# Attention and two mixture-of-experts layers in one kernel: other routing one-hots and ranks, one table of rows, another order of the attention loads

## The reference

```python
# attention: B 4, H 8, S 768, D 64; block 32, window 16
k_sum = k.reshape(B, H, nb, block, D).max(axis=3)
v_sum = v.reshape(B, H, nb, block, D).mean(axis=3)
scores_l = scale * q @ k^T         # kept where |i - j| < 16
scores_s = scale * q @ k_sum^T + log(32)
a = softmax(concat(scores_l, scores_s))
attn = a @ concat(v, v_sum)        # -> x: 3072 tokens of 512
# first expert layer: 8 experts, 512 -> 1024 -> 512
do = x @ w_skip > 0                # the others pass unchanged
e = argmax(x @ w_gate);  g = softmax prob of e
x[do] += g * (relu(x @ w1[e]) @ w2[e])
# second expert layer: the same sizes, each expert takes exactly 384 tokens
# all (token, expert) logits in falling order: a pair is taken if the token
# is free and the expert has room
out[mask_e] = relu(x[mask_e] @ w1[e]) @ w2[e]
```

## Time and profile before

| | us |
|---|---|
| median of 3 runs | 919.61 (914.32 to 926.02) |
| the profiled execution itself | 920.52 |
| its span, first to last instruction | 918.8 |
| mean granted TensorE clock | 0.920 |

### The profile page before, as it was taken

The page is one execution under the profiler, slowest core; times in us unless marked ns, Lnnn a source line. Parts: engine busy times, 40 slices in busy tenths (PEclk is TensorE's granted clock), DMA queues, the critical chain, the costliest instruction groups (busy, mean ns, idle before and its releaser), DMA issues.

```text
span 918.8 us, 14353 instructions
## 1 busy us (share of the span) xinstructions
PE 769.8 (84%) x4727; PEld 524.7 (57%) x4727; DVE 388.0 (42%) x1530; ACT 220.5 (24%) x685; POOL 185.6 (20%) x236
## 2 busy tenths in 40 slices
PE   2788888877079999994329999999999999999995
PEld 1788888877057777682225454454545545555552
DVE  4585767845602121113763636346363553620000
ACT  2666667754001111010001011110111101111110
POOL 4472736323021111111010020111101011031101
PEclk8898999989579999997558999999999999999998
DMA  8999795999073518600050330504205050155000
GB/s 187 201 244 227 183 244 129 244 254 293 13 280 130 194 58 322 246 7 7 1 218 1 126 127 1 218 34 164 88 10 208 35 218 35 53 220 197 35 0 34
DMA packets 137827, 126.02 MB, mean 137 GB/s; under 512 B 100722, under 2 KB 100722, under 8 KB 137584
## 3 DMA queue, kind: packets, MB, share of 16 engines
q1 hardware_dynamic: 125584, 94.74, 34.1%
q10 hardware_dynamic: 6432, 14.73, 5.6%
q0 software_dynamic: 5760, 15.87, 4.6%
HBM read 105.80 MB, written 22.74 MB: 140 GB/s over the span
## 4 chain that ended last, share of the span: by engine, by line
PE 66%; DVE 10%; DMA 9%; issue 5%; POOL 5%; SPq 2%; ACT 1%; POOLq 1%; DVEq 0%; ACTq 0%
PE bank L1085 19%; PE bank L1098 13%; PE bank L978 8%; PE bank L993 8%; DMA scratch<-rows_b,idx 4%; PE bank L1026 3%; DMA weights<-in_k 3%; PE bank L868 3%; PE bank L847 2%; POOL weights L626 2%; PE bank L1046 1%; PE bank L1058 1%; PE bank L857 1%; POOL scratch L657 1%; PE bank L890 1%
## 5 line engine op out<-in xcount | busy, mean ns | idle before, releaser
L1085 PE MATMUL bank<-scratch,weights 128*128 128x384 f32 x512 | 183.6, 503 | 0.7 <-ACT scratch L1261 0.7
L1098 PE MATMUL bank<-weights,scratch 128*128 128x512 f32 x384 | 178.8, 610 | 5.0 <-issue 2.5
L1085 PEld LDWEIGHTS bank<-scratch,weights 128*128 128x128 f32 x512 | 94.2, 192 | 59.7 <-issue 5.8
L1098 PEld LDWEIGHTS bank<-weights,scratch 128*128 128x128 f32 x384 | 70.3, 193 | 79.2 <-issue 76.4
L1167 ACT ACTIVATE scratch<-shared,neg_max 128x120 f32<-128x120 f32 x192 | 73.4, 383 | 45.6 <-DVE neg_max L1316 30.9
L1267 ACT ACTIVATE scratch<-bank 128x384 f32<-128x384 f32 x64 | 31.4, 490 | 171.1 <-PE bank L1085 171.1
L657 POOL TENSOR_TENSOR scratch<-scratch,row_inv 128x480 f32<-128x480 f32 x48 | 47.3, 986 | 99.2 <-DVE row_inv L1326 98.5
L978 PEld LDWEIGHTS bank<-mix,weights 128*128 128x128 f32 x512 | 60.6, 196 | 4.6 <-issue 4.6
L978 PE MATMUL bank<-mix,weights 128*128 128x128 f32 x512 | 61.5, 279 | 0.9 <-DVE mix L1522 0.9
L868 PE MATMUL bank<-shared,mix 120*128 120x128 f32 x384 | 53.2, 283 | 6.3 <-issue 6.3
L993 PE MATMUL bank<-weights,mix 128*128 128x512 f32 x128 | 58.4, 599 | 0.0
(11 more groups left out here) (234 smaller groups left out, 971.0 us busy)
## 6 DMA issues: line engine op xcount, KB each, us to landing
weights<-in_moe_w SPq DMA_DIRECT2D x20, 2048.0 KB, 11.6
scratch<-in_moe_w SPq DMA_DIRECT2D x8, 2048.0 KB, 15.6
weights<-in_moe_w ACTq DMA_DIRECT2D x16, 512.0 KB, 6.6
mix<-in_v SPq DMA_DIRECT2D x40, 192.0 KB
rows_a<-row SPq DMA_DIRECT2D x24, 260.5 KB, 4.1
rows_b<-row SPq DMA_DIRECT2D x24, 260.0 KB, 4.4
weights<-in_k SPq DMA_DIRECT2D x24, 256.0 KB, 5.6
scratch<-in_q SPq DMA_DIRECT2D x24, 256.0 KB, 4.8
```

Of the source, the lines that this page charges most:

```text
L1085: last = mm(hb2[f % 2][:, 0:CAP], w1_sb[odd][:, c, f * P:(f + 1) * P], xT2[odd][:, c, :], start=(c == 0), stop=(c == C - 1), skip_group_ch ...
L1098: last = mm(yb2[c % 2][:, :], hT2[odd][:, f, c * P:(c + 1) * P], w2_sb[odd][:, f, :], start=(f == 0), stop=(f == FC - 1), skip_group_check ...
```

## The change

- Each key tile has a semaphore of its own in every batch. SP's opening order is another: queries 3 after the first queries are turned and ahead of the means; the key tiles of batch 1 between windows. Keys of batch b + 2 are issued in tile steps 2, 3, 4, 4, 5, 5 of batch b.
- In odd steps the key turn follows the scores.
- The block means of batch 0: group 0 in five halvings on DVE after the key maxima, group 1 on POOL. In later batches POOL's fold starts a step earlier, its first halving is split over two steps, and the value block pieces are issued in steps 6 to 13 of the batch two before (before: 4 to 11).
- The quarters of the weights are issued in steps 39 to 46, one per step.
- One table `rows` of 529 columns (8 logits, 512 values, 9 logits) takes the place of both.
- First routing: tiles 0 to 22 are judged before the last tile's logits are copied; ranks over tiles come from 25 accumulating products; all one-hots have 16-bit operands and the tile index innermost. POOL loads one bound instead of nine and issues the first gather from the list itself.
- Second routing: the tokens of the closing expert are found from smaller operands, the updates of scores and assignments move behind the list's operands, the row one-hot is laid out in pairs of tiles, and `spacing` is another.

```diff
-            sp.wait_ge(s.v_sum_out, 16)
-            load_means(0)
-            load_means(1)
-            for g in range(2, VR, 2):
-                load_k(1, g - 2)
-                load_k(1, g - 1)
-                load_window(g)
-                load_means(g)
-                load_window(g + 1)
-                load_means(g + 1)
-            sp.wait_ge(s.q_turned, 1)
-            load_queries(3)
-            for j in range(TB - 2, TB):
-                load_k(1, j)
+            load_k(1, 0)
+            load_window(2)
+            sp.wait_ge(s.q_turned, 1)
+            load_queries(3)
+            sp.wait_ge(s.v_sum_out, 16)
+            for g in range(3):
+                load_means(g)
+            load_k(1, 1)
+            for g in range(3, VR):
+                load_window(g)
+                load_means(g)
+                load_k(1, g - 1)
+            load_k(1, TB - 1)
...
                 if b + 2 < B:
-                    sp.wait_ge(s.k_turned, TB * (b + 1))
-                    load_k(b + 2, w)
+                    for j in ((), (), (0,), (1,), (2, 3), (4, 5))[w]:
+                        sp.wait_ge(s.k_turned, TB * b + j + 1)
+                        load_k(b + 2, j)
...
+            FOLDS = 5
+            pool.wait_ge(s.blocks_in0, 16)
+            for step in range(FOLDS):
+                fold(0, step, slice(1, 2))
+            average(0, slice(1, 2))
             edges(0)
...
-                    at_ = n - (5 if b == 0 else 4)
+                    at_ = n - (4 if b == 0 else 3)
                     if at_ == 0:
                         pool.wait_ge(blocks_in[(b + 1) % 2], blocks_count(b + 1))
-                        fold(b + 1, 0)
+                        fold(b + 1, 0, slice(0, 1))
                     elif at_ == 1:
-                        fold(b + 1, 1)
-                        fold(b + 1, 2)
+                        fold(b + 1, 0, slice(1, 2))
                     elif at_ == 2:
-                        fold(b + 1, 3)
-                        fold(b + 1, 4)
-                        average(b + 1)
+                        fold(b + 1, 1, slice(0, 2))
                     elif at_ == 3:
+                        for step in range(2, FOLDS):
+                            fold(b + 1, step, slice(0, 2))
+                        average(b + 1, slice(0, 2))
...
-            mm(ranks[:, 0:NT * E], before[:, :], chosen_h.rearrange("p j e -> p (j e)"), start=True, stop=True)
-            mm(sums[:, 0:NT * E], ones[:, :], chosen_h.rearrange("p j e -> p (j e)"), start=True,
-               stop=True).then_inc(s.ranked_ps, 1)
+            mm(ranks[:, 0:(NT + 1) * E], before[:, :], chosen_h.rearrange("p j e -> p (j e)"), start=True, stop=False,
+               skip_group_check=True)
+            for j in range(NT):
+                last = mm(ranks[:, (j + 1) * E:(NT + 1) * E].rearrange("p (j e) -> p j e", e=E), ones[:, :],
+                          chosen_h[:, j:j + 1, :].to_broadcast([P, NT - j, E]), start=False,
+                          stop=(j == NT - 1), skip_group_check=True)
...
-                        last = mm(tot[:, 96:96 + 2 * CT], row_hot[:, :, j],
+                        last = mm(tot[:, 96:96 + 2 * CT], row_hot[:, j // 2, :, j % 2],
...
-            spacing = [20, 5, 10, 5] + [14, 5] * (ROUNDS - 2) + [13, 13, 11, 20]
+            spacing = [18, 7, 8, 7] + [12, 8] * (ROUNDS - 2) + [15, 11, 8, 17]
...
+                after = g - PIECES_AT          # 6
+                if 0 <= after and after // NH + 2 < B and after % NH < PIECES:
...
+                if QUARTERS_AT <= g < QUARTERS_AT + 2 * C:          # 39
...
-                v_.tensor_tensor(out=low_hot, in0=iota_row[:, :].rearrange("p (o n) -> p o n", o=1).to_broadcast([P, NT, P]),
-                                 in1=lo_f.rearrange("p (j o) -> p j o", o=1).to_broadcast([P, NT, P]), op=ALU.is_equal)
+                wide = [P, P, NT]
+                v_.tensor_tensor(out=low_hot, in0=iota_low[:, :, :],
+                                 in1=lo_h.rearrange("p (o j) -> p o j", o=1).to_broadcast(wide), op=ALU.is_equal)
...
+            link(judge(0, NT - 1))
+            copy_logits(NT - 1)
+            judge(NT - 1, NT).then_inc(s.phase_ready, 1)
+            copy_gates(NT - 1)
+            v_.memset(tile_bounds[:, 0:1], 0)
+            dve.wait_ge(s.ranked_ps, 1)
...
-                plink(v_.scalar_tensor_tensor(out=scores2, in0=over_experts(taken), ...
-                plink(v_.tensor_tensor(out=assigned, in0=assigned, in1=hot, op=ALU.add))
-                list_tokens(plink, ph, last_e)
+                plink(v_.tensor_tensor(out=mine_h, in0=taken, in1=here_h, op=ALU.mult))
+                plink(v_.tensor_tensor(out=mine_h, in0=mine_h, in1=kept_h, op=ALU.add))
...
+                list_tokens(plink, ph, update)
```

More of the change, by code:

```diff
@@ L262, in build @@
         first = sb("first", [P, NT])[:, :]
-        chosen = part(NT, E)
-        chosen_h = part(NT, E, dt=BF16)
-        prefix = part(NT, E)
-        tile_sum = [part(NT, E) for _ in range(2)]
-        count = part(E)
+        chosen_h = part(NT + 1, E, dt=BF16)
         over = part(E, NT)
@@ L392, in build @@
         at[0] = 0
-        xg2 = [part(CT, BROW) for _ in range(2)]
+        xg2 = [part(CT, ROW) for _ in range(2)]
         xT2 = [part(C, CAP) for _ in range(2)]
@@ L616, in _, with fold @@
             nc.gpsimd.memset(masks[:, 2, WK - WINDOW:WK], -1e30).then_inc(s.masks_made, 1)
-            v_links = [2]
-            def fold(b, step):
+            v_links = [0]
+            def fold(b, step, groups):
                 x = v_blocks[b % 2]
@@ L625, in fold @@
                 for lo in range(0, half, piece):
-                    last = nc.gpsimd.tensor_tensor(out=x[0:HB, :, lo:lo + piece], in0=x[0:HB, :, lo:lo + piece],
-                                                   in1=x[0:HB, :, half + lo:half + lo + piece], op=ALU.add)
+                    last = nc.gpsimd.tensor_tensor(out=x[0:HB, groups, lo:lo + piece], in0=x[0:HB, groups, lo:lo + piece],
+                                                   in1=x[0:HB, groups, half + lo:half + lo + piece], op=ALU.add)
                 last.then_inc(s.v_chain, 1)
@@ L902, in _ @@
                 kk = prepared(g)
-                if kk is not None:
+                if kk is not None and g % 2 == 0:
+                    pe.wait_ge(s.kT_vector, k_vector(kk))
+                    pe.wait_ge(s.kT_scalar, k_scalar(kk))
+                    turn_k(kk, kx)
+                if g + 2 < HT:
+                    score(g + 2)
+                if kk is not None and g % 2 == 1:
                     pe.wait_ge(s.kT_vector, k_vector(kk))
@@ L1383, in _ @@
             for g in range(HT + 2):
-                kk = prepared(g)
-                if kk is not None and kk % 2 == 0:
-                    put_k(kk, bank[7])
                 if g + 2 < HT:
@@ L1392, in _ @@
                     put_pT(g)
+                kk = prepared(g)
+                if kk is not None and kk % 2 == 0:
+                    put_k(kk, bank[7])
                 if 1 <= g <= HT:
@@ L1436, in running @@
                 return bufs[cur]
-            ranks, sums, table = bank[0], bank[1], bank[2]
-            def places(wait):
-                dve.wait_ge(s.ranked_ps, wait)
-                t3 = "p (j e) -> p j e"
-                link(v_.tensor_copy(tile_sum[0], sums[:, 0:NT * E].rearrange(t3, e=E)))
-                incl = running(link, tile_sum, NT, lambda x, a_, b_: x[:, a_:b_, :])
-                v_.tensor_copy(count, incl[:, NT - 1, :])
-                link(v_.tensor_tensor(out=place, in0=incl, in1=sums[:, 0:NT * E].rearrange(t3, e=E), op=ALU.subtract))
-                link(v_.tensor_tensor(out=place, in0=place, in1=ranks[:, 0:NT * E].rearrange(t3, e=E), op=ALU.add))
@@ new lines, in _, with judge @@
+            ranks, table = bank[0], bank[2]
+            def judge(a_, b_):
+                n = b_ - a_
+                experts = [P, n, E]
+                score = logits[:, a_:b_, 1:]
+                dve.wait_ge(s.logits_kept, b_)
+                v_.tensor_scalar(is_do[:, a_:b_], logits[:, a_:b_, 0], 0.0, None, ALU.is_gt)
+                link(v_.tensor_reduce(best[:, a_:b_], score, AX, ALU.max))
+                v_.tensor_scalar(none_at[:, a_:b_], is_do[:, a_:b_], -1.0, 4096.0, ALU.add, ALU.mult)
+                link(v_.tensor_tensor(out=equal[:, a_:b_, :], in0=score,
+                                      in1=best[:, a_:b_].rearrange("p (j o) -> p j o", o=1).to_broadcast(experts),
+                                      op=ALU.is_equal))
+                link(v_.tensor_tensor(out=equal[:, a_:b_, :], in0=equal[:, a_:b_, :],
+                                      in1=descend[:, :].rearrange("p (o e) -> p o e", o=1).to_broadcast(experts),
+                                      op=ALU.mult))
+                link(v_.tensor_reduce(first[:, a_:b_], equal[:, a_:b_, :], AX, ALU.max))
+                link(v_.tensor_tensor(out=equal[:, a_:b_, :], in0=equal[:, a_:b_, :],
```

(7 more changed lines are left out.)

276 lines of the change are left out of this document (136 added, 140 removed).

## The result

The changed kernel takes 887.55 us (median of four runs, 884.66 to 890.73); the kernel before takes 916.97 us beside it. The ratio is 0.9687, 95% interval [0.9641, 0.9734]: faster by 3.1%. The forecast was 880 in a range of 865 to 900. The profiled execution took 890.73 us (span 889.0) against 920.52 (918.8): 29.8 us less, where the sum of the steps had said 39.

A forecast was written before the change was run, and what follows sets the result against it. Attention was taken as bound by stalls, first routing by its instruction chain, second experts by TensorE's work and clock-losing idleness. 920.5 - 17 - 13 - 9 = 881.5, less 0.9 for the median: 880 us, range 865 to 900.

The forecast's parts named there:

- Start, -4: Attention's start: reductions split over DVE and POOL bring first scores to about 20.2 us from 25.3; constants +1; net -4 us.
- Keys to means, -2 and -3: Attention's batch changes: key stalls of 4.18 and 2.45 us vanish, most waiting moves to means; -2 and -3 us.
- Batch 3, -5.5: Attention's last batch: with weights starting at step 39 instead of 32, the 6.27 us stall shrinks to about 1; -5.5 us.
- Weights at the end, +2: Attention's end: 8 MB of weights issued in eight steps make rows and last windows slower; +2 us.
- Folds, -3: Attention's value-block folds on POOL: 4.66 us piece halved and spread, but later-issued blocks cause waits; -1 per batch, -3 us.
- First routing, -13: First routing: earlier judging, ranks by matmul, one scan, 16-bit one-hots, earlier gather; sum -13.5, taken as -13 us.
- Second routing, -9: Second routing and experts: shorter chain before list -0.8, faster list loads -6.4, earlier gathers -1.8; sum -9 us.
- 1 (strided read costs nothing): Second routing's list loads: cost set by columns alone, so -6.4 falls away; 887 us, chance 0.16.
- 2: Attention: each removed wait is replaced in the same full queues, only 4 of 17 us stay; 893 us, chance 0.14.
- 4: Attention's end and first routing: rows and first weights cause waits; -17 and -13 become -4 and -3; 903 us, chance 0.07.
- 3 (no clock losses): Second experts and attention: no stall lowers the clock (-9), means arrive in time (-5); 866 us, chance 0.09.
- 5, the spacing: Second routing: shorter flags-to-count window makes TensorE wait each round, lowering its clock; 935 us, chance 0.04.

The follow-up runs named there:

- both_pair: Changed kernel with both the loaded and the streamed operand of the first list laid out in pairs of tiles; ratio 0.9725 to the kernel before.
- consts_late: Changed kernel with POOL's 14 constants made one by one behind the scalings of windows 34 to 47, not before the first scaling; ratio 0.9709 to the kernel before.
- means_first: Changed kernel with SP issuing the four loads of means ahead of the two tiles of keys at a batch's last step; ratio 0.963 to the kernel before.
- weights_split: Changed kernel with the second expert's four quarters of weights loaded behind attention's last window instead of in windows 43 to 46; ratio 0.9665 to the kernel before.
- together: Changed kernel with means before keys, later weights, clearing held back, two register loads moved, first list paired from one constant table, second weight halves after gathers; 865.89 us.
- w2_later: Changed kernel with the second half of each second-routing expert's weights issued only when that expert's rows are gathered; ratio 0.9562 to the kernel before.
- update_first: Changed kernel with DVE's updates of scores, free tokens and assignments again ahead of each phase's list; ratio 0.9739 to the kernel before.
- low_pair: Changed kernel with only the loaded operand of the first list in pairs of tiles, the streamed one left at a step of 24; ratio 0.9666 to the kernel before.
- list_planes: Changed kernel with the second routing's row one-hot again laid out with the 24 tiles innermost; ratio 0.9668 to the kernel before.
- memset_bounds: Changed kernel with POOL's clearing held until the last judgement and three of TensorE's nine register loads moved behind the first token turning; ratio 0.967 to the kernel before.

## Why the prediction was right, and where it was not

The total fell inside the range because the range had room for attention's missing 7 us; of the terms, some failed and others made up for them.

**Start, -4.** Mis-sized. It was -5.1 for the first scores and +1 for two more constants. The scores came 3.75 us earlier (21.59, not 20.2), and TensorE's wait for POOL's first scaling grew from 1.57 to 3.69 us, +2.1; both_pair and consts_late show that POOL's row of constants sets it. Net -1.6. **Queries, -1.5.** The wait of 3.35 us went whole.

**Keys to means, -2 and -3.** Mis-sized. The mechanism was the forecast one (waits on means of 1 to 4 us), but 6.6 us of waits on keys became 7.2 us on means: nothing gained where I took 5. The row for it was there, 10.8 us from the first issue of means to their use in batch 3, against two steps of 4 us that the new order leaves: 2.8 us late at each change even without two tiles of keys ahead of the means, and I still booked a gain. (That row was read beside the load of the weights; with the means first, 1.1 to 1.3 us of waiting are left at each change.) means_first shows what stood there: 4.8 us less of these two waits, and last gates 8.4 us earlier, of which some may be the scatter between executions.

**Batch 3, -5.5.** The 6.27 us are gone. **Weights at the end, +2.** Mis-sized: stores landing after 14 us held ACT 5.55 and 2.56 us, and weights_split puts the last gates 4.5 us earlier. I had spread 8 MB over eight steps and not asked which small transfer lies behind them with someone waiting. **Folds, -3.** Not tested by itself, but the size agrees: TensorE's waits behind POOL's scalings in attention, without the first, sum to 5.4 us instead of 8.1, and two of 1.4 us (at 108.90 and 158.10 in the kernel before) have no counterpart.

**First routing, -13.** By its own terms: last gates to ranks 6.4 to 2.9 us (-3.5, forecast -3.3); ranks 4.0 to 2.4 (-1.6, -1.6); scan, one-hots and small ones 10.8 to 6.9 (-3.9, -4.0); products and list 2.7 to 4.1 (+1.4, +0.4); list to turned tokens 10.3 to 6.3 (-4.0, -5). The +0.4 failed in kind: I priced the strided load, and it was the strided streamed operand. The -5 was mis-sized: TensorE turns the tokens 6.3 us behind the list, after its nine loads, where I had taken POOL's 5.3.

**Second routing, -9.** Right in sum, wrong in its main term. The load is as forecast (33 ns a product instead of 73; 38 was taken, -0.8 a list), and it is worth next to nothing: with the old layout the run is as fast. The step that failed is "-0.8 for each of eight lists, **-6.4**": it took work off TensorE that TensorE then waits out, in turn2 and at L1047, or pays back with the clock in the sixth expert. I had credited turn2's waits with 1.8 us and not asked what ends them. What the stage cannot do without is the late update: undone, it costs 9 to 10 us in the profiled executions, phase 0 included. I had counted it in phase 0 alone because "DVE works beside the products". Two things hang on DVE's chain: the issue of the weights, with the rows behind them, and, under the new distances, a step of TensorE's own. That the total of this stage came out at 9.0 is luck.

The Trainium skill's rule ("TensorE: Matmul & The Clock Gate", section "Weight-path perf modes": columns packed or strided alike) does not hold for the loads here, 33 ns a product with a step of 2 elements against 73 with 24. By it the stage was to give 2.6 us. It gave 9.0, and the difference has nothing to do with the rule.

**Rivals.** 1 (strided read costs nothing) is refuted for the load; its run, 887 us, is what was measured, but for other reasons. 2 and 4, attention giving its gain back, came half: 7 us of 17. 3 (no clock losses) came with together, after other edits, and with w2_later but for its first expert. 5, the spacing, was not seen in the rounds (its comparison with the gain used 39.5 us where the sum has 39); the new distances do cost 2.5 us, in the sixth expert, by making TensorE early for a gather.

## What to carry to other kernels

Before work is taken off an engine, find what ends its next wait, and follow that back to where it is issued: five instructions of DVE ahead of a 4 MB issue cost 9 us of the stage in the trace (part of it by a wait of TensorE's own), while 8 us of TensorE's work behind that issue were worth nothing. Where a small transfer that someone needs soon and a large one that nobody needs yet are issued together, let the large one wait: that gave 8 us for means, 4 for rows and 9 for gathers here, the first two by the ends of attention in single traces, the last clear in the run too. And price a strided layout for both operands, the streamed one above all.

## What the runs showed of the hardware

A gather of three times 128 rows landed 6.5 us after POOL's first issue with half of the weights ahead of it (w2_later), and 8.6 to 9.0 with all 4 MB under way (changed kernel and update_first; 380 GB/s from 606 to 619 us). "DMA: Bandwidth & Descriptors" of the Trainium skill, section "Queues, rings and completion order", has the DMA engines rotate between their queues by packets; the trace agrees in so far as the gather is slowed and not shut out: issued 6.1 us behind the weights, the rows are there by 619.88, and the second half of the weights, issued at 605.60, takes 14.4 us to land in the median.

At half clock, 24 products of 128 loaded and 68 streamed bf16 columns took 1.54 us with both operands at a step of 2 elements (both_pair), 3.08 with the streamed one at 24 (low_pair), and 3.20 with both (changed kernel). With 6 streamed columns at full clock the load decides: 0.78 us at a step of 2, 1.75 at 24 (list_planes).

An iota of 816 elements a partition took 0.98 us as 34 runs of 24, and 4.80 us as 408 runs of 2; one of 3072 as 128 runs of 24 took 3.32, and 256 as 128 runs of 2 took 1.53. Here it is the short runs that cost: an element in a run of 2 took 6 ns, in a run of 24 1.1 to 1.2.

A DVE instruction of 0.17 us took 1.42 and 2.14 us when it was issued during POOL's memset of 3.12 us, and ended 0.04 us after it both times; with the memset held back it took 0.17 again (memset_bounds).
